# An eight-stage kernel on one core: fewer idle products in the last batch, squares in another place of ScalarE's list, own PSUM places for the last chunk

## The chip, the core and the metric

The kernel runs on one core of a Trainium2 chip. The core has a matrix engine (TensorE, PE in the profile), a vector engine (VectorE, DVE), a scalar engine (ScalarE, ACT), GpSimd (POOL), and SyncE (SP), which here only starts transfers (DMA) between HBM and SBUF. Each engine works through its own list of instructions in order; semaphores make one wait for another. The matrix engine writes to PSUM, which has 8 banks of 512 float32 for each of 128 partitions. The metric is the time of one execution on the device in microseconds; lower is better.

## What is computed

Cut to what matters:

```python
for t in range(S):                       # attention: B=4, H=8, S=768, D=48
    new_re = ar * S_re - ai * S_im       # a = (a_re, a_im), scaled to magnitude <= 0.999
    new_im = ar * S_im + ai * S_re
    S_re, S_im = new_re + outer(k[t], v[t]), new_im
    y[t] = q[t] @ S_re
x = y as [3072, 384]
logits = x @ phi                         # soft mixture of experts, 8 experts x 4 slots
d = softmax over tokens;  slot_input = d.T @ x
slot_out[e] = relu(slot_input[e] @ w1[e]) @ w2[e]
x = softmax over slots(logits) @ slot_out
out = relu(x @ w_in)**2 @ w_out          # second feed-forward, 2048 wide
```

## The kernel before

The recurrence is worked chunk by chunk: a batch has NC = 6 chunks of 128 steps, B = 4 batches, NT = 24 chunks. For a whole batch VectorE builds the running products of the decays `a` in the tile `big` (a scan: L798, L800, L804, then three block steps that end with L827, its copy L811 ahead of each). ScalarE and VectorE first bring `a` to its magnitude: squares (L381, L382), logarithms and exponentials, `inv_mag` (L404), `bend` (L410), then VectorE's `normalise` (L772). ScalarE's `sign_planes` (L448, L449, L451) makes negated copies of the imaginary plane; the scan of a batch opens with `init_products` (L782), which waits for the semaphores `signed` and `an_ready`. Behind the scan ScalarE takes the squares of the products (`product_squares`, L420, in two parts), VectorE adds them (`square_sums`, L833), and ScalarE makes logarithms and exponentials of them between two table loads (L430, L426, L433, L439).

For each chunk n VectorE makes weighted keys and queries (`key_query`, L894; `weigh`, L876) and a turn matrix (`build_turn`, L906); SyncE stacks them with six transfers (L269) into `stk`. On the matrix engine, iteration n of the main loop (the last lines of the kernel) runs: `scores(n)` (L1127), for every second n `flip` (L1207) of a pair of chunks, `outputs(n-1)` (L1167, L1170), `flip`, `next_state(n)` (L1145, L1148), `weighted_sums` of the pair (L1216, L1220), `turn_x(n-1)` (L1196), `logits(n-1)` (L1184). Between them stand idle products: `keep_busy(count)` (L1113) multiplies the identity into partitions 96 to 127 of PSUM bank 7, which nobody reads. VectorE masks the scores (`apply_mask`, L915), ScalarE copies results out of PSUM: `copy_kt` (L458), `copy_state` (L464), `copy_y` (L470), `copy_raw` (L477), `copy_x` (L485), the exponentials of a pair (L491, L497, L499), `copy_flipped` (L507), `copy_sums` (L511).

What sets the order: every engine's list is written out by hand. ScalarE's loop runs over batches p and chunks c; iteration (p, c) does the copies for chunk n = 6(p-1)+c and, between them, the preparation of batch p+1 (`inv_mag`, `bend` at c = 4, table loads and signs at c = 5). VectorE's loop has the same shape; `go` and `fill` put steps of the next batch's scan between the steps of the chunks. So iterations c = 4 and c = 5 are where a batch hands over to the next: "the hand-over" below. From chunk 18 on there is no next batch to prepare. Chunk 23 is the last; after it come the last pair's exponentials, flips and weighted sums, and then the experts (L1264 on) and the feed-forward (L1367 to L1397), 96 rounds that take the second half of the time. The experts' weights (`wt`) are loaded in halves by ScalarE's queue (L366, L372) and whole by SyncE's (L284, L290).

PSUM: scores fill banks 0 to 3, `s_ps` (states) and `lgt_ps` (logits) lie in bank 4, `y_ps` (outputs) in bank 5, `x_ps` and the flips in bank 6, the sums in bank 7.

## Time and profile before

| what | us |
|---|---|
| median of 3 runs | 618.05 |
| lowest, highest | 617.24, 618.3 |
| profiled execution, its time | 617.78 |
| its span (first to last instruction) | 616.1 |
| PE busy | 512.4 (83%) |
| VectorE busy | 392.4 (64%) |
| ScalarE busy | 339.4 (55%) |

The rows further down come from the profiled execution. Times in them are us from the start of its span. A row of a timeline gives start, length, engine, line of the kernel, operation, what is written from what, shapes, and in square brackets how long the engine sat idle before it and what released it. Rows of one line that follow one another are merged (x3); matmuls overlap, so the length of a matmul row is longer than the distance to the next row.

### The profile page before, as it was taken

What the parts mean: (1) busy time and instruction counts of PE and PEld (TensorE: products, weight loads), DVE (VectorE), ACT (ScalarE), POOL (GpSimd) and SP (SyncE); (2) the same over time, 40 slices, a digit from 0 to 9 for tenths busy, and PEclk for the clock granted to TensorE, in tenths of its full rate; (3) what the DMA queues carried; (4) which work ended last, traced back from release to release, by engine and by line L of the source; (5) the groups of instructions that cost most, each with busy time, mean ns of one, the idle gap of its engine ahead of it and who ended that gap; (6) DMA issues with size and microseconds to landing.
All of it is one profiled execution on the core that took longest, in us unless ns stands there. A gap on an engine that the chain in (4) does not pass through costs nothing.

```text
span 616.1 us, 11719 instructions
## 1 busy us (share of the span) xinstructions
PE 512.4 (83%) x4566; PEld 386.4 (63%) x4566; DVE 392.4 (64%) x649; ACT 339.4 (55%) x593; POOL 138.4 (22%) x118
## 2 busy tenths in 40 slices
PE   1000459995998869997999999999999999999997
PEld 1000147774667646775788644578888888888886
DVE  5899999979999799995353151599423333233322
ACT  6818714697456953375243412676655555555653
POOL 7000000000000000000000000266555555555553
PEclk9655589997999979997999999999999999999999
DMA  7400575647655358886799999200101001010101
GB/s 272 153 1 0 113 207 129 146 93 193 170 119 147 71 152 205 231 210 145 190 278 257 422 426 421 99 1 2 53 0 53 0 1 51 2 51 2 53 0 52
DMA packets 41319, 79.59 MB, mean 129 GB/s; under 512 B 7344, under 2 KB 28976, under 8 KB 40112
## 3 DMA queue, kind: packets, MB, share of 16 engines
q1 hardware_dynamic: 39104, 67.44, 38.3%
q10 hardware_dynamic: 2160, 11.40, 5.3%
q8 instruction: 36, 0.59, 0.4%
q14 instruction: 19, 0.16, 0.1%
HBM read 55.12 MB, written 4.72 MB: 97 GB/s over the span
## 4 chain that ended last, share of the span: by engine, by line
PE 61%; DVE 24%; ACT 5%; issue 5%; DMA 3%; SPq 2%; DVEq 0%; ACTq 0%
PE ps L1397 10%; PE ps L1393 10%; PE ps L1394 10%; PE ps L1127 7%; PE ps L1113 4%; DVE tt L798 4%; PE ps L1367 3%; DVE big L772 3%; DVE tt L800 3%; DVE big L804 3%; PE ps L1184 2%; PE ps L1170 2%; DMA stk<-xout 2%; PE ps L1167 2%; PE ps L1287 2%
## 5 line engine op out<-in xcount | busy, mean ns | idle before, releaser
L1092 DVE TENSOR_TENSOR qs<-rs 128x512 f32<-128x512 f32 x96 | 82.7, 861 | 118.8 <-ACT rs L674 118.8
L735 POOL TENSOR_TENSOR hlo<-qs,hhi 128x512 fp32r<-128x512 f32 x96 | 126.1, 1313 | 125.0 <-DVE qs L1092 119.8
L1113 PE MATMUL ps<-ident 128*32 128x512 bf16 x274 | 81.3, 408 | 52.7 <-DVE xout L894 52.7
L1393 PE MATMUL ps<-hhi,who 128*128 128x512 f32 x285 | 110.9, 389 | 0.0
L1394 PE MATMUL ps<-hhi,wlo 128*128 128x512 f32 x285 | 110.9, 389 | 0.0
L674 ACT ACTIVATE rs<-ps 128x512 f32<-128x512 f32 x96 | 57.4, 598 | 82.2 <-PE ps L1367 82.1
L1127 PE MATMUL ps<-stk 112*128 112x224 f32 (+1 forms) x384 | 77.8, 358 | 12.7 <-DMA stk<-xout 12.7
L1127 PEld LDWEIGHTS ps<-stk 112*128 112x128 f32 x384 | 69.5, 199 | 23.9 <-DMA stk<-xout 18.3
L1397 PE MATMUL ps<-hlo,who 128*128 128x512 f32 x285 | 80.5, 391 | 0.1
L727 POOL MEMSET sinz<- 128x768 f32 x1 | 0.7, 738 | 335.9 <-PE ps L1170 335.9
L1113 PEld LDWEIGHTS ps<-ident 128*32 128x32 bf16 x274 | 23.0, 100 | 77.7 <-DVE xout L894 53.0
L678 ACT ACTIVATE hhi<-rs 128x512 fp32r<-128x512 f32 x96 | 60.8, 633 | 3.1
L1397 PEld LDWEIGHTS ps<-hlo,who 128*128 128x128 f32 x285 | 53.2, 188 | 12.2 <-POOL hlo L735 1.3
L1393 PEld LDWEIGHTS ps<-hhi,who 128*128 128x128 f32 x285 | 53.5, 188 | 11.2
L1394 PEld LDWEIGHTS ps<-hhi,wlo 128*128 128x128 f32 x285 | 53.5, 188 | 11.1
L915 DVE TENSOR_TENSOR asb<-ps,mask 128x512 f32<-128x512 f32 x48 | 32.5, 686 | 28.7 <-ACT kts L458 14.5
L458 ACT ACTIVATE kts<-ps 128x384 f32<-128x384 f32 x40 | 19.5, 487 | 52.4 <-PE ps L1127 52.4
L894 DVE TENSOR_TENSOR xout<-big,xq 128x768 f32<-128x768 f32 x48 | 45.7, 953 | 0.5
L1367 PE MATMUL ps<-cst,ust 128*128 128x512 f32 x96 | 37.4, 392 | 0.2 <-DVE ust L1074 0.2
L1170 PE MATMUL ps<-asb,vr 128*48 128x128 f32 x384 | 35.5, 273 | 0.0
L1167 PE MATMUL ps<-stk,st 112*48 112x128 f32 x320 | 31.8, 276 | 0.0
L1184 PE MATMUL ps<-xts,phs 112*32 112x128 f32 x576 | 28.3, 294 | 3.4 <-issue 2.9
(152 smaller groups left out, 795.5 us busy)
## 6 DMA issues: line engine op xcount, KB each, us to landing
stk<-xout SPq DMA_DIRECT2D x144, 128.0 KB, 3.7
wt<-in_w SPq DMA_DIRECT2D x8, 1536.0 KB, 15.2
wt<-in_w ACTq DMA_DIRECT2D x14, 768.0 KB, 6.1
big<-in_a_all SPq DMA_DIRECT2D x12, 768.0 KB, 5.5
xq<-in_xq SPq DMA_DIRECT2D x24, 384.0 KB, 4.2
vr<-in_v_all SPq DMA_DIRECT2D x24, 192.0 KB, 4.1
out<-ost SPq DMA_DIRECT2D x5, 768.0 KB, 3.5
wins<-in_w_in SPq DMA_DIRECT2D x1, 3072.0 KB, 19.8
```

The source lines that it names most:

```text
L674: nc.scalar.activation(rs[:, i % NQS, :], ps[:, i % 2, :], ACT.Relu).then_inc(relu_ready, 1)
L678: nc.scalar.activation(hhi[:, i % NHS, :], rs[:, i % NQS, :], ACT.Square).then_inc(hi_ready, 1)
L735: pool.tensor_tensor(hlo[:, i % NHS, :], qs[:, i % NQS, :], hhi[:, i % NHS, :].bitcast(F32), ALU.subtract).then_inc(lo_ready, 1)
L894: dve.tensor_tensor(o, e, x, ALU.mult).then_inc(kq_ready, 1)
L1092: dve.tensor_tensor(qs[:, i % NQS, :], rs[:, i % NQS, :], rs[:, i % NQS, :], ALU.mult).then_inc(sq_ready, 1)
L1113: nc.tensor.matmul(ps[P - SL:P, bank, :], idb[:, 0:SL], idle, start=True, stop=True)
L1127: last = nc.tensor.matmul(ps[:, h // 2, h % 2 * SK:h % 2 * SK + cols], x[:, 0:CH], x[:, CH:CH + cols], start=True, stop=True)
L1170: last = nc.tensor.matmul(y, vr[:, n % NV, h * D:(h + 1) * D], asb[:, n % 2, h], start=(c == 0), stop=True)
L1367: nc.tensor.matmul(ps[:, i % 2, :], ust[:, f * P:(f + 1) * P], cst[:, t * TW:(t + 1) * TW], start=True, stop=True).then_inc(g_done, 1)
L1393: nc.tensor.matmul(accs[k], wh[k], hi, start=(f == 0), stop=False)
L1394: nc.tensor.matmul(accs[k], wl[k], hi, start=False, stop=False)
L1397: last = nc.tensor.matmul(accs[k], wh[k], lo, start=False, stop=(f == F2B - 1))
```

## The change

It has five parts, two of them small.

1. Idle products. In iterations 19 to 23 of the matrix engine's loop the idle products before `scores`, `outputs`, `weighted_sums` and `turn_x` are gone (5 + 5 + 3 + 5 = 18 products); iteration 18 keeps its 20 before `scores` and one before the others.
2. Squares and masks, for the hand-overs after batch preparation 0, 1 and 2 (p < 3). On ScalarE at c = 4 the first part's squares stand where `inv_mag` and `bend` stood, ahead of the pair's exponentials; `inv_mag`, the second part's squares and `bend` follow the copy of the state. On VectorE the first `square_sums` comes behind the masks of the chunk, not ahead of them (for p = 1 and 2).
3. The last chunk's outputs, logits, transpose and flips go to banks 0 to 3, which the masks have read by then. `outputs(23)` follows `outputs(22)` at once, both `logits` come before the last but one `weighted_sums`; the copy of the last outputs is split over ScalarE and VectorE, and VectorE takes over the copies of `x` for chunks 22 and 23 and of the sums of pair 10.
4. In the first batch the last third of `normalise` is split into the imaginary and the real half, and the signs wait for the imaginary half alone (`im_ready`).
5. Three quarters of the weight tile 6 are loaded at chunks 1, 3 and 5 of p = 2 by ScalarE's queue, the last quarter at chunk 18, in place of two halves at chunks 18 and 19.

```diff
-        et_ps = [ps[:, 6, NU * XR:NU * XR + 2 * SL]] * (NT - 1) + [ps[:, 4, 0:2 * SL]]
+        et_ps = [ps[:, 6, NU * XR:NU * XR + 2 * SL]] * (NT - 2) + [ps[:, 3, 0:2 * SL], ps[:, 4, 0:2 * SL]]
...
+        last_y = ps[:, 0, :].rearrange("p (u t) -> p u t", u=NU)
+        last_lgt = ps[0:SR, 1, 0:CH]
+        last_x = ps[:, 2, 0:NU * XR].rearrange("p (u r) -> p u r", u=NU)
...
-        LOADED = [48 if k == 5 else 32 if k in EARLY + [10] else 16 for k in range(2 * NX)]
+        LOADED = [64 if k == 6 else 48 if k == 5 else 32 if k in EARLY + [10] else 16 for k in range(2 * NX)]
...
             def sign_planes(b, t):
-                act.wait_ge(an_ready, DT * b + t + 1)
+                if b == 0 and t == DT - 1:
+                    act.wait_ge(im_ready, 1)
+                else:
+                    act.wait_ge(an_ready, DT * b + t + 1)
                 if b and t == 0:
...
                 act.wait_ge(y_done, m + 1)
                 if m >= 2:
                     act.wait_ge(x_done, m - 1)
+                if m == NT - 1:
+
+                    nc.scalar.activation(xts[0:D, m % 2], last_y[0:D], ACT.Copy).then_inc(last_y_copied, 1)
+                    return
                 nc.scalar.activation(xts[:, m % 2], y_ps, ACT.Copy).then_inc(y_copied, 1)
...
@@ -538,6 +551,9 @@
             for p in range(B + 1):
                 for c in range(NC + 2 * (p == B)):
                     n = (p - 1) * NC + c
+                    if p == B - 2 and c % 2:
+
+                        load_part(6, c // 2, c // 2 + 1)
...
                             magnitude(p + 1, 1)
                             log_mag(p + 1, 0)
                         elif c == 4:
-                            for t in range(DT):
-                                inv_mag(p + 1, t)
-                            for t in range(DT):
-                                bend(p + 1, t)
+                            product_squares(p, 0, 0)
+                            product_squares(p, 0, 1)
...
                             act.wait_ge(kq_ready, 2 * NC * (B - 1))
-                        load_half(NC + c)
+                        if c == 0:
+                            load_part(6, 3, 4)
+                        if c >= 2:
+                            load_half(NC + c)
...
                             magnitude(p + 1, 2)
                             log_mag(p + 1, 1)
-                    if p < B and c == NC - 2:
-
-                        product_squares(p, int(p == B - 1), 0)
-                        product_squares(p, int(p == B - 1), 1)
+                    if p == B - 1 and c == NC - 2:
+
+                        product_squares(p, 1, 0)
+                        product_squares(p, 1, 1)
...
@@ -614,19 +631,22 @@
                         elif c == 3:
                             log_mag(p + 1, 2)
                         elif c == 4:
+                            for t in range(DT):
+                                inv_mag(p + 1, t)
                             product_squares(p, 1, 0)
                             product_squares(p, 1, 1)
-                    if pair is not None:
+                            for t in range(DT):
+                                bend(p + 1, t)
+                    if pair is not None and n != NT - 1:
                         copy_sums(pair)
                     if p == B - 1 and c == NC - 2:
                         exponential(p, 0, 1)
                     if n == NT - 1:
                         copy_y(n)
-                    if n == NT:
-                        copy_raw(n - 1)
+
+                    if 1 <= n < NT - 1:
+                        copy_x(n - 1)
                     if 1 <= n <= NT:
-                        copy_x(n - 1)
-                    if 1 <= n < NT:
                         copy_raw(n - 1)
...
+                if b == 0 and t == DT - 1:
+
+                    for c, done in ((1, im_ready), (0, an_ready)):
+                        dve.scalar_tensor_tensor(out=grid(PL[0] + c * PF + t * PT, [1, PT]), in0=grid(U_ + t * PT, [1, PT]),
+                                                 scalar=KNEE, in1=grid(RAW + c * PF + t * PT, [1, PT]), op0=ALU.subtract,
+                                                 op1=ALU.mult, reverse0=True).then_inc(done, 1)
+                    return
...
-                    if 0 < p < B and c == NC - 1:
+                    if p == B - 1 and c == NC - 1:
 
                         one(p)
...
+            def last_copy_y():
+
+                dve.wait_ge(y_done, NT)
+                dve.wait_ge(x_done, NT - 2)
+                dve.tensor_copy(xts[R1:R1 + D, (NT - 1) % 2], last_y[R1:R1 + D]).then_inc(last_y_copied, 1)
...
+            def last_copy_x(m):
+                dve.wait_ge(x_done, m + 1)
...
+                x = bass.AP(ps, x.offset, [list(x.ap[0]), [XR, NU], [R1, 2], [1, D]])
+                dve.tensor_copy(xsb[:, m % NX3, 0:DM].rearrange("p (u r e) -> p u r e", u=NU, r=2), x).then_inc(x_copied, 1)
+
+            def last_copy_sums(j):
+                dve.wait_ge(sums_done, j + 1)
+                dve.tensor_copy(sums[0:SR, :], sums_ps).then_inc(sums_copied, 1)
+
+            last_copy_y()
             running_max(NT // 2 - 1)
+            last_copy_sums(NT // 2 - 2)
+            for m in (NT - 2, NT - 1):
+                last_copy_x(m)
...
-                if n:
+                if 0 < n < NT - 1:
...
             def logits(m):
 
-                pe.wait_ge(y_copied, m + 1)
+                if m == NT - 1:
+                    pe.wait_ge(last_y_copied, 2)
+                else:
+                    pe.wait_ge(y_copied, m + 1)
                 pe.wait_ge(s_copied, turns(min(m + 2, NT)))
-                if m:
+                if m == NT - 1:
+                    pe.wait_ge(masked, 2 * NT)
+                elif m:
                     pe.wait_ge(raw_copied, m)
...
-                pe.wait_ge(y_copied, m + 1)
-                if m:
+                if m == NT - 1:
+                    pe.wait_ge(last_y_copied, 2)
+                else:
+                    pe.wait_ge(y_copied, m + 1)
+                if m == NT - 1:
+                    pe.wait_ge(masked, 2 * NT)
+                elif m:
                     pe.wait_ge(x_copied, m)
...
                 pe.wait_ge(exp_done, m // 2 + 1)
-                pe.wait_ge(x_copied, m // 2 * 2 + (2 if m >= NT - 4 else 3))
-                if m == NT - 1:
+                if m < NT - 2:
+                    pe.wait_ge(x_copied, m // 2 * 2 + (2 if m >= NT - 4 else 3))
+                if m == NT - 2:
+                    pe.wait_ge(masked, 2 * NT)
+                elif m == NT - 1:
                     pe.wait_ge(raw_copied, NT)
...
                 full = n < NT - NC
+
+                rest = int(n <= NT - NC or n >= NT)
                 pair = pair_at(n)
                 if n < NT:
                     if n:
-                        keep_busy(20 if n == NT - NC else 6 if full else 1)
+                        keep_busy(20 if n == NT - NC else 6 if full else 0)
                     scores(n)
                 if pair is not None:
                     flip(2 * pair)
                 if 1 <= n < NT:
-                    keep_busy(1)
+                    keep_busy(rest)
                     outputs(n - 1)
+                if n == NT - 1:
+                    outputs(n)
                 if pair is not None:
                     flip(2 * pair + 1)
                 if n < NT and has_turn(n):
                     keep_busy(2 if full else 0)
                     next_state(n)
+                if n == NT - 1:
+
+                    logits(n - 1)
+                    logits(n)
                 if pair is not None:
-                    keep_busy(1)
+                    keep_busy(rest)
                     weighted_sums(pair)
-                if n == NT - 1:
-                    outputs(n)
-                if n == NT:
-                    logits(n - 1)
                 if 1 <= n <= NT:
-                    keep_busy(2 if full else 1)
+                    keep_busy(2 if full else rest)
                     turn_x(n - 1)
-                if 1 <= n < NT:
+                if 1 <= n < NT - 1:
                     logits(n - 1)
```

ScalarE's list at the first hand-over with chunks in flight (p = 1, c = 4; chunk 4). Before, from the reciprocals of the magnitudes to the copy of the sums:

```order
L404 ACTIVATE big<-big 128x768 x3
L410 ACTIVATE big<-big 128x768 x3
L491 ACTIVATE eb<-eb 32x256
L458 ACTIVATE kts<-ps 128x384
L507 ACTIVATE lgx<-ps 128x2x32
L458 ACTIVATE kts<-ps 128x384
L420 ACTIVATE big<-big 128x6x288 x2
L470 ACTIVATE xts<-ps 128x512
L507 ACTIVATE lgx<-ps 128x2x32
L464 ACTIVATE st<-ps 112x384
L420 ACTIVATE big<-big 128x6x96 x2
L511 ACTIVATE sums<-ps 96x385
```

and now (L425 is the squares, L409 `inv_mag`, L415 `bend`, L466 `copy_kt`, L482 `copy_y`, L472 `copy_state`, L504 the exponentials, L524 the sums):

```order
L425 ACTIVATE big<-big 128x6x288 x2
L504 ACTIVATE eb<-eb 32x256
L466 ACTIVATE kts<-ps 128x384
L520 ACTIVATE lgx<-ps 128x2x32
L466 ACTIVATE kts<-ps 128x384
L482 ACTIVATE xts<-ps 128x512
L520 ACTIVATE lgx<-ps 128x2x32
L472 ACTIVATE st<-ps 112x384
L409 ACTIVATE big<-big 128x768 x3
L425 ACTIVATE big<-big 128x6x96 x2
L415 ACTIVATE big<-big 128x768 x3
L524 ACTIVATE sums<-ps 96x385
```

The three L404 and three L410 have moved from ahead of the exponentials to behind the copy of the state; the squares L420 on 288 columns have moved the other way.

The matrix engine's list from the scores of chunk 23 to the last weighted sums. Before, from the outputs of chunk 23 on (L1167 and L1170 alternate above the first row, too):

```order
L1170 MATMUL ps<-asb,vr 48x128 x2
L1113 MATMUL ps<-ident 32x512
L1196 MATMUL ps<-ident,xts 128x112 x4
L1184 MATMUL ps<-xts,phs 32x128 x24
L1113 MATMUL ps<-ident 32x512
L1196 MATMUL ps<-ident,xts 128x112 x4
L1207 MATMUL ps<-ident,eb 128x64 x2
L1113 MATMUL ps<-ident 32x512
L1216 MATMUL ps<-sums,scale_diag 32x385
L1220 MATMUL ps<-xsb,lgx 32x385 x2
```

and now, from the flip that follows the outputs of chunk 23 (L1238 is the logits, L1255 the transpose of `x`, L1162 the idle product, L1269 the flip, L1278 and L1282 the weighted sums):

```order
L1269 MATMUL ps<-ident,eb 128x64
L1238 MATMUL ps<-xts,phs 32x128 x24
L1278 MATMUL ps<-sums,scale_diag 32x385
L1282 MATMUL ps<-xsb,lgx 32x385 x2
L1255 MATMUL ps<-ident,xts 128x112 x4
L1162 MATMUL ps<-ident 32x512
L1255 MATMUL ps<-ident,xts 128x112 x4
L1269 MATMUL ps<-ident,eb 128x64 x2
L1162 MATMUL ps<-ident 32x512
L1278 MATMUL ps<-sums,scale_diag 32x385
L1282 MATMUL ps<-xsb,lgx 32x385 x2
```

The logits of both chunks now stand ahead of a weighted sum that used to stand ahead of the outputs of chunk 23, and the two flips of the last pair stand behind the transpose of chunk 23 as before.

VectorE's list behind the last masks, now (L1050, L1061 and L1057 are new on this engine; L948 is the running maximum, which stood alone before):

```order
L942 TENSOR_TENSOR asb<-ps,mask 128x512 x2
L1050 COPY xts<-ps 48x512
L948 TENSOR_REDUCE eb<-eb 96x1
L1061 COPY sums<-ps 96x385
L1057 COPY xsb<-ps 128x384 x2
```

Behind it the three copies stand in a row, one to each of the sums and the two `x`.

## Rows read from the trace of the kernel before

**Rows 1.** Windows: length, then PE, PEld, DVE, ACT, POOL busy (x count), granted clock, DMA share, GB/s.

```profile
146.00:148.00 2.00, 1.32 (x10) 1.02 (x13) 1.93 (x5) 0.90 (x3) 0.00 (x0) 0.50 0.84 199
296.00:341.00 45.00, 45.00 (x695) 37.16 (x694) 19.53 (x27) 17.90 (x45) 0.00 (x0) 1.00 0.92 252
```

**Rows 2.** Timeline of ScalarE, hand-over from batch 1 to 2 (p = 1, chunks 4, 5).

```profile
122.51 2.30 ACT L404 ACTIVATE big<-big 128x768 f32<-128x768 f32 x3
...
126.91 0.49 ACT L491 ACTIVATE eb<-eb 32x256 f32<-32x256 f32 x1
...
128.26 3.18 ACT L420 ACTIVATE big<-big 128x1728 f32<-128x1728 f32 x2
...
132.31 0.49 ACT L464 ACTIVATE st<-ps 112x384 f32<-112x384 f32 x1 [0.27 <-PE ps L1148]
132.70 1.25 ACT L420 ACTIVATE big<-big 128x576 f32<-128x576 f32 x2
133.84 0.47 ACT L511 ACTIVATE sums<-ps 96x385 f32<-96x385 f32 x1
...
143.92 0.52 ACT L451 ACTIVATE big<-big 128x384 f32<-128x384 f32 x1
```

**Rows 3.** Timeline of VectorE, same hand-over.

```profile
131.47 1.96 DVE L833 TENSOR_TENSOR big<-big 128x1728 f32<-128x1728 f32 x1 [3.66 <-ACT big L420]
...
144.70 0.18 DVE L782 COPY a<-big 128x36 f32<-128x36 f32 x1
```

**Rows 4.** Timeline of the matrix engine, same hand-over.

```profile
127.46 0.27 PE L1207 MATMUL ps<-ident,eb 64*128 64x64 f32 x1 [1.07 <-ACT eb L491]
...
146.68 1.01 PE L1196 MATMUL ps<-ident,xts 112*128 112x112 f32 x4 [6.50 <-ACT xts L470]
...
151.06 3.29 PE L1127 MATMUL ps<-stk 112*128 112x224 f32 x16 [0.44 <-DMA stk<-xout]
```

**Rows 5.** Timelines of ScalarE and VectorE, hand-over from batch 2 to 3.

```profile
217.72 0.52 ACT L451 ACTIVATE big<-big 128x384 f32<-128x384 f32 x1
...
218.64 0.18 DVE L782 COPY a<-big 128x36 f32<-128x36 f32 x1
```

**Rows 6.** Timelines of ScalarE and VectorE, first batch and its hand-over.

```profile
21.73 0.52 ACT L448 ACTIVATE big<-big 128x384 f32<-128x384 f32 x1 [0.16 <-DVE big L772]
...
55.07 3.18 ACT L420 ACTIVATE big<-big 128x1728 f32<-128x1728 f32 x2 [0.40 <-DVE big L827]
...
60.75 1.28 ACT L430 ACT_TABLE_LOAD   x1
...
69.74 0.53 ACT L451 ACTIVATE big<-big 128x384 f32<-128x384 f32 x1
...
71.39 0.18 DVE L782 COPY a<-big 128x36 f32<-128x36 f32 x1
```

**Rows 7.** Timeline of the matrix engine in the last batch, around two idle products.

```profile
304.17 0.39 PE L1113 MATMUL ps<-ident 128*32 128x512 bf16 x1
304.26 0.50 PE L1184 MATMUL ps<-xts,phs 112*32 112x128 f32 x9
...
307.92 0.39 PE L1113 MATMUL ps<-ident 128*32 128x512 bf16 x1
308.24 1.08 PE L1170 MATMUL ps<-asb,vr 128*48 128x128 f32 x16
```

**Rows 8.** Timelines of the matrix engine and ScalarE, the last chunk's end.

```profile
342.99 0.39 PE L1113 MATMUL ps<-ident 128*32 128x512 bf16 x1
...
346.85 0.43 PE L1167 MATMUL ps<-stk,st 112*48 112x128 f32 x4
...
354.31 0.48 PE L1216 MATMUL ps<-sums,scale_diag 96*32 96x385 f32 x1
...
348.87 0.60 ACT L470 ACTIVATE xts<-ps 128x512 f32<-128x512 f32 x1 [1.42 <-PE ps L1170]
...
352.27 0.28 ACT L477 ACTIVATE eb<-ps 96x128 f32<-96x128 f32 x1 [1.26 <-PE ps L1184]
```

16 lines of the change are left out of this document (10 added, 6 removed).

## The prediction

> **What bounds the kernel now.** I read first the windows of the trace by stage, then the timelines of the three engines at the places where the diff edits a list, each time asking which wait ends last. Three kinds of stretch matter.
>
> In the last batch the matrix engine is the bound: from 296 to 341 it is busy 45.00 of 45.00 us, with a granted clock of 1.00 (2.4 GHz) [rows 1]. What is taken from its list there comes off the time, as long as nothing else is late next.
>
> At a hand-over between batches it is idle: 6.50 us pass before the transposes at 146.68, released by ScalarE's copy of the outputs (L470) [rows 4]. ScalarE is the engine to follow here. From 122.51 its list runs without a gap to speak of: reciprocals and bends, the pair's exponentials at 126.91, the squares at 128.26, the state at 132.31 after 0.27 idle, more squares, the sums at 133.84, and, through the two table loads, to the last sign at 143.92 [rows 2]. VectorE waits 3.66 us for the squares in the middle (L833), and that also holds the masks behind it; but it opens the next scan (L782, which needs all signs) at 144.70, when the last sign ended at 144.44 [rows 2, 3]. So both engines come out at the same moment, and whichever gets longer decides.
>
> Inside batches 1 to 3 VectorE's scan sets the pace (scores wait for the stack transfer of what VectorE made: 0.44 us at 151.06 [rows 4]). A scan that opens later shifts the whole batch behind it, because every wait of the matrix engine, ScalarE's copies and VectorE's masks hangs on the same transfers.
>
> **The squares and masks, ScalarE's side.** The edit swaps what ScalarE does in two of its waiting times. Before: 4.40 us of reciprocals and bends (122.51 to 126.91) lie beside the scores, and the 3.1 us of first squares lie beside the outputs of chunk 3. Now the squares lie beside the scores, from 122.51 to 125.6; their input, the second block step, was done before. Nothing at all lies beside the outputs and the next state, and the 4.40 us come behind the state copy. Step by step at the hand-over 1 to 2:
>
> The flip started at 127.46 because the exponentials were late, after 1.07 us of idling [rows 4]. Now it comes some 1.15 us earlier (the idle time plus an end of a modelled product), and so do outputs and next state. The state copy, which waited for next state until 132.31 [rows 2], starts at 131.16 and takes the 0.39 up to the squares, until 131.55. Then 4.40 of reciprocals and bends and 1.14 of second squares (132.70 to 133.84) follow: the sums start at 131.55 + 4.40 + 1.14 = 137.09, not at 133.84. ScalarE is 3.25 us late. It has bought 1.15 us and lost some 4.4 us of cover. From there its list is as before, so the last sign ends at 147.7.
>
> **The same place, VectorE's side.** The wait of 3.66 us goes [rows 3]. What is late next: the first sum no longer waits, but the second needs the second squares, which end at 134.9 by the working above (137.09 less the bends, half of 4.40). Keys and queries of the next batch could come at most 2.5 us earlier (3.66 less some 1.2 for the masks that now stand first); with the wait for the second squares I estimate 0.9. `weigh` then needs an exponential that ScalarE makes 3.2 us later, and L782 needs the signs: 147.7 against 144.70, so **+3.0 us** for the scan (3.25 less the 0.26 between 144.44 and 144.70). The transposes behind L470 are 3.2 us late as well; there the 0.44 us of idle before the scores of chunk 6 is used up first, +2.8 [rows 4]. The scan's figure is the larger, and it carries through the batch.
>
> Hand-over 2 to 3 is the same list one batch on. The last sign ended at 218.24, L782 ran at 218.64 [rows 5], so 0.40 of ScalarE's 3.2 is hidden: **+2.8**.
>
> Hand-over 0 to 1 has no chunks in flight. ScalarE had finished the bends and waited 0.40 us for the second block step until 55.07 [rows 6]. Now it has nothing to do before that. From 54.9 (0.16 earlier, see below) it does squares 3.1, reciprocals and bends 4.40, second squares 1.14, and reaches the table load at 63.5, not 60.75: 2.75 late. The signs end at 73.0, not 70.27, and L782 had run at 71.39 [rows 6]: **+1.6**.
>
> Sum of part two: 1.6 + 3.0 + 2.8 = **+7.4 us**. Its lower bound is a gain, if ScalarE's lateness never reached VectorE: twice the 0.9 above. Its upper bound is 2.75 + 3.25 + 3.2 = 9.2. I take the working, because L782's wait for the signs is in the code and both sides of it have their rows.
>
> **First batch.** The last signs started at 21.73, only 0.16 us after ScalarE had become free [rows 6]. Whatever the half-sized `normalise` gains, 0.16 is all that ScalarE can use. It is counted above (54.9), with nothing to add.
>
> **Idle products, 18 of them.** Their price is not one number. Before the outputs one costs 0.32 us, from 307.92 to 308.24 [rows 7]; iterations 19 to 22 lose one each there, and a product after another kind of product needs some start of its own, so I take 0.30: 1.2 us. Before scores it costs nothing: at 304.17 it starts ahead of the last nine logits at 304.26 [rows 7], since it writes partitions 96 to 127 and they write 0 to 95. The weighted sums write 0 to 95 as well, so I count nothing there and nothing for the transpose behind them. That leaves the transposes of iterations 19 and 21; the logits behind these also wait for the state copy, which is late next, so 0.2 each, 0.4. Sum **-1.6** (bounds: -1.0, and 18 times 0.32, -5.8; I stay near the low end, since eight of the rows' kind are hidden).
>
> The Trainium skill ("TensorE: Matmul & The Clock Gate", Part 3, on row and column tiling) says that small products at different tile positions overlap in the array but start and end strictly in program order. By the second half an idle product queued behind the logits could not start before the last of them, and would cost its own length each time, some 0.2 us for eight of them, 1.6 us more gain. The first row of [rows 7] stands ahead of the second, which speaks for the overlap and against that price.
>
> **The last chunk.** Outputs of chunk 23 started at 346.85. Now they follow those of chunk 22, which can start at 342.99, where an idle product stood, and take about 1.8: 344.8. The copy that ran at 348.87 would run at 346.8, but on ScalarE the flipped pair's copy now comes between: 347.1, done at 347.7. Before, the copy of the last logits followed 3.40 us after it (348.87 to 352.27); now only the 1 us of logits(23) lies between: 348.85. From there to the last weighted sums it was 2.04 us (352.27 to 354.31), which would give 350.9 [rows 8]. But other things end later: the matrix engine still has a weighted sum, two transposes and an idle product to do (about 2.2 us, until 350.9), and VectorE's last `x` copy waits for the second transpose and ends near 351.6. So 354.31 becomes 351.6: **-2.7**. Its bounds: -2.0 (the outputs' shift alone) and -3.4 (350.9). No row shows VectorE copying 48 or 96 partitions from PSUM; the nearest is ScalarE's 0.60 for 512 columns [rows 8]. From 0.3 to 0.7 each, three in a row, moves the end by 0.6 either way.
>
> **Weight tile 6.** It adds three issues on ScalarE's queue in batch 2, none on a path that waits. Their transfers share the DMA engines with the stacks that scores wait for. At 199 GB/s [rows 1] 384 KB is 2.0 us; if the stacks of two chunks stood behind one each, that is 4.0, and it is 0 if the slack ahead of the masks takes it. I take **+0.2**. In the last batch it takes load off the DMA engines, share 0.92 [rows 1], and the matrix engine shows no wait there that it could give back: 0.
>
> **Sum.** 7.4 + 0.2 - 1.6 - 2.7 = **+3.3 us**. The profiled execution took 617.78, 0.27 below the median of the runs; laid on the median, 618.05 + 3.3 = 621.35, **621.3 us**. The experts and the feed-forward behind this are as before.
>
> **Rivals.**
> (a) The masks are the path, and ScalarE's lateness is not (the scan opens late, but VectorE has room). Then part two gives 2 x 0.9 back and the time is 618.05 - 1.8 - 1.6 - 2.7 + 0.2 = 612.2. For it: the 3.66 us wait [rows 3]. Against: 144.44 beside 144.70 [rows 2, 3]. It decides if ScalarE's late list stays under 0.26 us. Chance 0.10.
> (b) The scan opens late, but half of it is given back in the batches, because the matrix engine and not VectorE sets some chunks' pace: 3.7 in place of 7.4, 617.65. Chance 0.18. For it: the wait at 151.06 is just 0.44.
> (c) The last chunk gains nothing, since VectorE's three copies, one behind the other, take the place of the removed waits: 623.9. Chance 0.08.
> (d) Without idle products the matrix engine pauses in the last batch and its clock falls. After the 6.50 us pause the granted clock was 0.50 (1.2 GHz), and four transposes lasted 1.01 us [rows 1, 4]. Against: nothing else but useful products is left in a stretch without idle time, and the new waits are tenths. If a quarter of the 45 us came to run at half clock, it would take 11 us more: 632. Chance 0.03. The Trainium skill (same page, Part 1, on what is happening) has the throttled state as the default that activity releases, which is the rule against removing idle products; it can bite only where real products do not fill the time.
>
> **Chances and range.** The forecast has 0.61, and (a) to (d) 0.39. What a measurement of this kernel can tell from no change is about 0.2%, 1.2 us. The forecast's own spread is 619 to 623.5, and about 0.05 of its 0.61 falls within 0.2%; of (b), 0.10 falls within and 0.08 below. Slower: 0.56 + 0.08 + 0.03 = 0.67; within: 0.15; faster: 0.18. The range has to take in (b) and (c): 616.3 to 624.4.
>
> **What would show it.** Right: ScalarE idles 1.5 us twice between the second `copy_kt` and the state copy of chunks 4 and 10; the copy that opens each scan (now L809) waits for signs at all three hand-overs; the matrix engine idles some 10 us before the transposes of chunk 4, not 6.50; from scores(19) to the last weighted sums 4.3 us less. Wrong: VectorE's scan of batch 2 opening at or before 144.7 (then (a)), a first scores of batch 3 shifted by less than half of the sum (then (b)), a granted clock under 1.00 after chunk 19 (then (d)).

## The result and the profile after

| | before | changed |
|---|---|---|
| median of 6 runs, us | 617.30 | 621.54 |
| lowest, highest | 616.49, 618.30 | 620.57, 625.29 |
| profiled execution, its span | 617.78, 616.1 | 620.58, 618.8 |

The ratio is 1.0074, with a 95% interval of 1.0046 to 1.0103: the changed kernel is slower, by 4.2 us in the medians and by 2.8 us between the two profiled executions. The forecast was 621.3. It fell on the measured number, but two of its terms were wrong and offset each other, as the experiments show. (The ratios leave out executions over 1.5% above the fastest of the same kernel; the medians are of all, so the two can differ a little.)

Code lines have moved: L782 is now L809, L833 L860, L420 L425, L404 L409, L410 L415, L451 L459, L470 L482, L1127 L1176, L1167 L1216, L1196 L1255.

**Hand-overs.** ScalarE of the changed kernel, hand-over 1 to 2 (start, length, engine, line; in brackets the idle time before, and who ended it); answers [rows 2]:

```profile
123.94 3.17 ACT L425 ACTIVATE big<-big 128x1728 f32<-128x1728 f32 x2
...
130.28 0.60 ACT L482 ACTIVATE xts<-ps 128x512 f32<-128x512 f32 x1 [1.62 <-PE ps L1219]
...
132.59 0.49 ACT L472 ACTIVATE st<-ps 112x384 f32<-112x384 f32 x1 [1.60 <-PE ps L1197]
132.98 2.30 ACT L409 ACTIVATE big<-big 128x768 f32<-128x768 f32 x3
135.18 1.24 ACT L425 ACTIVATE big<-big 128x576 f32<-128x576 f32 x2
136.32 2.30 ACT L415 ACTIVATE big<-big 128x768 f32<-128x768 f32 x3
138.52 0.47 ACT L524 ACTIVATE sums<-ps 96x385 f32<-96x385 f32 x1
...
148.53 0.52 ACT L459 ACTIVATE big<-big 128x384 f32<-128x384 f32 x1
```

The squares now lie beside the scores, and ScalarE then stands idle 1.62 and 1.60 us for the matrix engine with nothing left to put there. Reciprocals and bends come behind. The sums start at 138.52, 4.68 later than at 133.84 [rows 2]; 1.43 of that the batch brought along (its chunk 4 started that much later), so 3.25 were made here.

VectorE of the changed kernel, same hand-over and the two others; answers [rows 3, 5, 6]:

```profile
72.91 0.18 DVE L809 COPY a<-big 128x36 f32<-128x36 f32 x1 [1.72 <-ACT big L459]
...
136.45 0.76 DVE L860 TENSOR_TENSOR big<-big 128x576 f32<-128x576 f32 x1 [2.87 <-ACT big L425]
...
149.08 0.18 DVE L809 COPY a<-big 128x36 f32<-128x36 f32 x1 [1.72 <-ACT big L459]
...
225.40 0.18 DVE L809 COPY a<-big 128x36 f32<-128x36 f32 x1 [1.72 <-ACT big L459]
```

The wait of 3.66 us ahead of the first sum became one of 2.87 ahead of the second, and each scan opens behind a wait of 1.72 us for signs. Against 71.39, 144.70 and 218.64 [rows 3, 5, 6] the scans open 1.52, 4.38 and 6.76 us later. Before the transposes of a hand-over the matrix engine now waits longer, here from batch 2 to 3, where it was 6.49 us (10.82 at the hand-over 1 to 2, where it was 6.50 [rows 4]):

```profile
227.61 1.01 PE L1255 MATMUL ps<-ident,xts 112*128 112x112 f32 x4 [10.83 <-ACT xts L482]
```

**Last batch.** Windows from one chunk's first scores to the next one's, chunks 18 to 22 (length, then PE, PEld, DVE, ACT, POOL busy, granted clock, DMA share, GB/s), of the changed kernel; they answer the second of [rows 1]:

```profile
301.59:310.61 9.02, 9.02 (x121) 7.17 (x120) 4.54 (x6) 3.27 (x8) 0.00 (x0) 1.00 0.70 170
310.61:317.99 7.38, 7.28 (x127) 6.57 (x124) 4.54 (x7) 2.83 (x6) 0.00 (x0) 1.00 0.98 247
317.99:328.69 10.70, 9.50 (x152) 7.80 (x149) 5.38 (x8) 4.72 (x13) 0.00 (x0) 1.00 0.84 219
328.69:336.95 8.26, 8.16 (x140) 7.45 (x140) 3.68 (x5) 2.56 (x5) 0.00 (x0) 1.00 0.75 221
336.95:346.37 9.42, 9.42 (x151) 7.80 (x148) 1.38 (x2) 4.45 (x12) 0.00 (x0) 1.00 0.94 299
```

The same stretches of the kernel before:

```profile
295.67:304.69 9.02, 9.02 (x121) 7.17 (x120) 4.55 (x6) 3.28 (x8) 0.00 (x0) 1.00 0.62 181
304.69:312.54 7.85, 7.85 (x130) 6.72 (x127) 4.96 (x7) 2.83 (x6) 0.00 (x0) 1.00 0.98 262
312.54:322.33 9.79, 9.79 (x155) 7.89 (x153) 4.55 (x6) 4.45 (x12) 0.00 (x0) 1.00 1.07 268
322.33:331.06 8.73, 8.73 (x146) 7.61 (x143) 4.09 (x6) 2.83 (x6) 0.00 (x0) 1.00 1.00 254
331.06:340.81 9.75, 9.75 (x156) 7.90 (x153) 1.38 (x2) 4.45 (x12) 0.00 (x0) 1.00 0.91 285
```

Read the second column of times, PE busy: without idle products a chunk from 19 on needs 0.57, 0.29, 0.57 and 0.33 less. The length shrinks by 0.47, 0.47 and 0.33 in chunks 19, 21 and 22, but it grows by 0.91 in chunk 20, where 1.20 us of the window is no work at all:

```profile
328.69 1.59 PE L1176 MATMUL ps<-stk 112*128 112x224 f32 x7 [1.20 <-DMA stk<-xout]
```

The scores of chunk 21 wait for their stack to land. I had not foreseen this wait. It also spoils one of the prediction's signs: from scores(19) to the last weighted sums it took 46.44 us, 49.62 before, 3.2 less and not 4.3. The last chunk came out as worked out, here the matrix engine's outputs(23) and last weighted sums, and ScalarE's copy of the last logits; answers [rows 8]:

```profile
350.35 0.39 PE L1216 MATMUL ps<-stk,st 112*48 112x128 f32 x4
...
357.05 0.51 PE L1278 MATMUL ps<-sums,scale_diag 96*32 96x385 f32 x1
...
354.42 0.27 ACT L489 ACTIVATE eb<-ps 96x128 f32<-96x128 f32 x1 [0.60 <-PE ps L1238]
```

**The sum in the trace.** Scan of batch 3 +6.76; scores of chunk 18 only +5.92 (0.84 given back on the way, see the clock below); scores of chunk 23 +5.56; last weighted sums 357.05 against 354.31 [rows 8], +2.74; the executions +2.80.

### The profile page after: what moved, and what is told of

It reads as the page before. It is cut to its first block, busy times and chain, and to the rows that moved or that the text cites. A ratio compares the mean times of both kernels' runs of the same rounds, so it can differ in the third digit from the quotient of the medians.

```text
span 618.8 us, 11687 instructions
## 1 busy us (share of the span) xinstructions
PE 506.3 (82%) x4548; PEld 384.7 (62%) x4548; DVE 395.1 (64%) x654; ACT 338.2 (55%) x590; POOL 138.5 (22%) x118
## 4 chain that ended last, share of the span: by engine, by line
PE 66%; DVE 13%; ACT 11%; DMA 4%; issue 4%; SPq 2%; ACTq 0%; DVEq 0%
PE ps L1463 11%; PE ps L1459 10%; PE ps L1460 10%; PE ps L1176 8%; PE ps L1162 5%; PE ps L1433 4%; DMA stk<-xout 3%; DVE tt L825 3%; DVE big L831 3%; DVE tt L827 3%; PE ps L1219 2%; PE ps L1216 2%; PE ps L1238 2%; SPq L274 2%; PE ps L1353 2%
## 5 line engine op out<-in xcount | busy, mean ns | idle before, releaser
L1162 PE MATMUL ps<-ident 128*32 128x512 bf16 x256 | 73.4, 404 | 52.4 <-DVE xout L921 52.4
L1176 PE MATMUL ps<-stk 112*128 112x224 f32 (+1 forms) x384 | 76.8, 355 | 16.6 <-DMA stk<-xout 16.6
L1176 PEld LDWEIGHTS ps<-stk 112*128 112x128 f32 x384 | 68.6, 196 | 27.3 <-DMA stk<-xout 20.7
L1162 PEld LDWEIGHTS ps<-ident 128*32 128x32 bf16 x256 | 21.2, 99 | 75.7 <-DVE xout L921 52.7
L466 ACT ACTIVATE kts<-ps 128x384 f32<-128x384 f32 x40 | 19.5, 487 | 49.8 <-PE ps L1176 49.8
L1255 PE MATMUL ps<-ident,xts 112*128 112x112 f32 x96 | 15.3, 284 | 21.8 <-ACT xts L482 21.8
L1216 PE MATMUL ps<-stk,st 112*48 112x128 f32 x320 | 31.8, 276 | 0.0
```

The costliest lines, as they stand in the source:

```text
L1162: nc.tensor.matmul(ps[P - SL:P, bank, :], idb[:, 0:SL], idle, start=True, stop=True)
L1176: last = nc.tensor.matmul(ps[:, h // 2, h % 2 * SK:h % 2 * SK + cols], x[:, 0:CH], x[:, CH:CH + cols], start=True, stop=True)
```

## Experiments

The five parts are called idle products, squares (with the masks), last chunk, normalise, and tile 6, as in the change. The runs of 1 to 4 shared the same runs of the kernel before (median 618.1), so did 5 to 8 (617.8) and 9 to 12 (618.6); each of these three groups ran on a chip of its own, so that ratios are compared between groups, and not medians. In these hours the kernel before spread from 613.8 to 627.7, so that intervals are some 0.3% to either side, and differences of 1 us are not settled. The diffs are cut to what matters.

**1. The changed kernel with the squares as before.** Against the changed kernel:

```diff
                         elif c == 4:
-                            product_squares(p, 0, 0)
-                            product_squares(p, 0, 1)
+                            for t in range(DT):
+                                inv_mag(p + 1, t)
+                            for t in range(DT):
+                                bend(p + 1, t)
...
-                    if p == B - 1 and c == NC - 2:
+                    if p < B and c == NC - 2:
...
-                    if p == B - 1 and c == NC - 1:
+                    if 0 < p < B and c == NC - 1:

                         one(p)
```

> The changed kernel with the squares and masks put back as they were (ScalarE's list at the hand-overs, VectorE's first sum of squares before the masks); idle products, last chunk, weight tile 6 and the halved normalise stay as changed. Theory (ScalarE's late list holds back the scan, 1.5 + 2.9 + 2.4 = 6.8 us in the trace of the changed kernel): the time falls from 621.5 to about 614.7, or to 615.7 if the 1.2 us that the changed kernel got back at the last hand-over goes too; scans 1 to 3 open at 71.4, 144.7 and 218.6 again, give or take 0.5. Rival (the new waits come from the other parts, the DMA traffic of weight tile 6 or the pauses without idle products, and the squares only move a wait): under 3 us of the 6.8 come back, the time stays above 618.5, and scans 2 and 3 open over 1.5 us later than in the kernel before.

Median 615.0, ratio to the kernel before 0.9931 (0.9899 to 0.9963). Scans 1 to 3 opened at 71.18, 145.22 and 218.98, within 0.52 of the kernel before. Against the changed kernel's 1.0074 this is 1.4% or about 9 us (6 to 11 with both intervals; the medians differ by 6.5). That agrees with the 6.8 expected, and not with the rival's 3. In the trace the third scan opened 6.42 us earlier than in the changed kernel. The rest of the change, on its own, gains.

**2. The kernel before with the squares alone.** The same lines as in experiment 1, the other way round, in the kernel before.

> The kernel before with the squares and masks alone moved. Theory: 617.3 + 6.8 = 624.1, the scans opening at 72.9, 149.1 and 225.4; 623.1 if the last hand-over gives back some 1.0 us as it did in the changed kernel. Rival (as for the run with the squares put back): under 620.

Median 626.5, ratio 1.0150 (1.0114 to 1.0185), 7.0 to 11.4 us. The scans opened at 73.39, 149.81 and 226.21, the last one 7.57 late. The profiled execution took 624.4, 6.6 more than that of before. The theory stands; the times show rather more than the trace.

**3. The kernel before with the last chunk alone.**

```diff
                 if 1 <= n < NT:
                     keep_busy(1)
                     outputs(n - 1)
+                if n == NT - 1:
+                    outputs(n)
...
+            last_copy_y()
             running_max(NT // 2 - 1)
+            last_copy_sums(NT // 2 - 2)
```

> The kernel before with the last chunk alone changed. Theory: the whole saving of 2.8 us between scores(23) and the last weighted sums belongs to this part: 614.5 (scan openings unchanged). Rival (it needs the free slots where the idle products stood, or VectorE's three new copies in a row take the gain): 615.8 or more.

Median 614.8, ratio 0.9965 (0.9940 to 0.9990), 0.6 to 3.7 us less. From the first scores of chunk 23 to the last row of weighted sums it took 11.35 us, 13.91 before: 2.56 gained (2.88 together with the idle products gone from these iterations). So the part works alone. The profiled execution took 618.45 all the same: it was 2.0 us ahead of the kernel before at scores(20) and 3.3 behind at scores(23). scores(21) had waited 3.54 us for its stack, and the chunk behind took 1.70 us longer than before. Its code up to there is that of the kernel before; why it waited is taken up behind the experiments.

**4. The kernel before without the 18 idle products.**

```diff
+                rest = int(n <= NT - NC or n >= NT)
...
-                        keep_busy(20 if n == NT - NC else 6 if full else 1)
+                        keep_busy(20 if n == NT - NC else 6 if full else 0)
...
-                    keep_busy(1)
+                    keep_busy(rest)
                     outputs(n - 1)
```

> The kernel before with 18 idle products of the last batch removed, nothing else. Theory (each removed one is worth 0.2 to 0.3 us where it stood before outputs or a transpose, nothing where it overlapped; 1.6 us in all, of which the changed kernel lost 1.2 to a stack transfer that chunk 21's scores then waited for): between 615.7 and 616.9, with a wait of the matrix engine for a stack transfer in the last batch if it is the upper figure. Rival 1 (idle products are never overlapped, each costs its own length): 3.2 us less, 614.1, and 2 us or more gained between scores(19) and scores(23). Rival 2 (the clock falls without them): granted clock under 1.00 after scores(19), 620 or more.

Median 621.9, ratio 1.0037 (0.9998 to 1.0075): no gain, and more likely a loss of some 2 us. My figure is out, and so is rival 1's. Rival 2 had named both the time and a lower clock, but the trace shows another cause than the one it gave. Matrix engine and windows of chunks 20 and 21:

```profile
323.23 4.98 PE L1127 MATMUL ps<-stk 112*128 112x224 f32 x16 [3.90 <-DMA stk<-xout]
```

```profile
309.85:323.23 13.38, 9.48 (x151) 7.79 (x149) 5.37 (x8) 4.72 (x13) 0.00 (x0) 1.00 1.08 248
323.23:333.19 9.96, 9.86 (x141) 8.82 (x141) 3.67 (x5) 2.56 (x5) 0.00 (x0) 0.83 0.57 168
```

The DMA engines are full in chunk 20 (share 1.08), scores(21) waits 3.90 us, and after that wait the granted clock of the next chunk is 0.83, with the scores at 4.98 us where they take 3.29 at full clock ([rows 4], third row). That chunk took 9.96 us, 1.70 more than the 8.26 of the changed kernel. Up to the wait the clock was 1.00 without the idle products, and experiment 3, which kept them, lost as much in the same place. So the product count was right (chunks 19 and 22 were 0.46 and 0.34 shorter), and 3.90 + 1.70 were lost between.

That is not all of this execution's loss. At the last weighted sums it was 1.45 us behind the kernel before, at its end 5.4: it lost 4.0 in the experts, where it ran at half the clock. Windows of experiment 4, then of the kernel before:

```profile
355.00:360.00 5.00, 4.43 (x22) 2.72 (x23) 0.30 (x2) 1.04 (x5) 0.00 (x0) 0.50 1.00 424
360.00:365.00 5.00, 5.00 (x28) 2.56 (x30) 3.92 (x8) 0.84 (x1) 0.29 (x1) 0.50 1.01 428
```

```profile
355.00:360.00 5.00, 4.42 (x39) 2.64 (x38) 2.62 (x5) 0.72 (x2) 0.29 (x1) 1.00 1.01 428
360.00:365.00 5.00, 5.00 (x49) 2.22 (x45) 3.18 (x6) 1.80 (x3) 0.00 (x0) 1.00 1.00 419
```

The code there is the same in both, and no run shows what set the clock there. In the traces of experiments 6 and 8 the clock fell in the same place too, for 1.7 us more; in the other eleven it stayed at 1.00. One execution therefore can't divide the 2 us of the medians among these causes.

**5. The changed kernel with tile 6 loaded as before.**

```diff
-                    if p == B - 2 and c % 2:
-
-                        load_part(6, c // 2, c // 2 + 1)
...
-                        if c == 0:
-                            load_part(6, 3, 4)
-                        if c >= 2:
-                            load_half(NC + c)
+                        load_half(NC + c)
```

> The changed kernel with weight tile 6 loaded as before (two halves in the last batch). The runs so far showed stack transfers as what the last batch waits for: scores(21) waited 3.5 and 3.9 us in the two kernels that had one part of the change without the moved weight tile, and 1.2 and 1.4 us in the two that had it moved; after a wait of 3.5 us or more the granted clock of the next chunk was 0.84, which cost 1.5 us more. New theory: the moved weight tile is worth some 3 to 4 us as soon as the matrix engine gets to scores(21) earlier, so here the time rises from 621.5 to 624.5 or more, with scores(21) waiting over 2.5 us for its stack and a granted clock under 0.9 in the chunk behind it. Rival (my forecast: its load costs 0.2 and saves nothing): 621.3, the wait at scores(21) stays near 1.2.

Median 625.7, ratio 1.0126 (1.0091 to 1.0161). The changed kernel had 1.0074: tile 6 moved is worth 0.5%, about 3 us (0.4 to 6), in this company. Matrix engine and windows of chunks 20 and 21:

```profile
333.18 6.26 PE L1170 MATMUL ps<-stk 112*128 112x224 f32 x16 [5.00 <-DMA stk<-xout]
```

```profile
318.69:333.18 14.49, 9.49 (x152) 7.80 (x149) 5.38 (x8) 4.72 (x13) 0.00 (x0) 0.97 1.09 238
333.18:344.42 11.24, 11.14 (x141) 9.74 (x141) 3.68 (x5) 2.56 (x5) 0.00 (x0) 0.73 0.42 134
```

Wait and clock are both there: 5.00 us where the changed kernel waited 1.20, then 0.73. The rival is out.

**6. The kernel before with tile 6 alone moved.** The lines of experiment 5, the other way round, in the kernel before.

> The kernel before with weight tile 6 alone moved. New theory: the median falls by 1 to 2 us, since some executions of the kernel before must pay the wait at scores(21) too (its times spread from 615 to 625), and the spread narrows; DMA share of the chunk ahead of scores(21) 0.85 in place of 1.07. My forecast's view: 0.2 slower.

Median 619.2, ratio 1.0023 (0.9993 to 1.0053). No gain by itself; the expectation was wrong. In the trace the relief is there (the stack lands 7.39 us after the start of scores(20), 9.74 before), but there is a price that I had missed. ScalarE of this kernel around the issue at chunk 7:

```profile
161.77 3.05 ACTq L372 DMA_DIRECT2D wt<-in_w  x1
164.93 0.84 ACT L381 ACTIVATE big<-big 128x768 f32<-128x768 f32 x1 [2.89 <-issue]
```

The issue took 3.05 us, where one takes 0.33 in the last batch, and nothing behind it on ScalarE's list can start. The copy of the outputs came 0.92 us later than before, but the scan of batch 3 opened only 0.18 later (218.82), so this trace doesn't show that the issue cost the kernel time.

**7. Last chunk, normalise and tile 6; squares as before, idle products kept.** Against experiment 1 it has `keep_busy(1)` where that has `keep_busy(rest)`, and 1 where that has 0:

```diff
-                        keep_busy(20 if n == NT - NC else 6 if full else 0)
+                        keep_busy(20 if n == NT - NC else 6 if full else 1)
...
-                    keep_busy(rest)
+                    keep_busy(1)
```

> The kernel with the last chunk, weight tile 6 and the halved normalise changed, the squares as before and the idle products of the last batch kept. It differs from the first experiment by the 18 idle products alone. New theory (with the stack transfer as the bound ahead of scores(21), a removed idle product only lengthens that wait; behind chunk 21 some 0.8 us are left): 0 to 0.8 us above the first experiment's time in the same hours, so 615.0 to 615.8. Rival (they are worth the 1.6 us of my sum): 616.6.

Median 613.4, ratio 0.9937 (0.9900 to 0.9973), against 615.0 and 0.9931 in experiment 1. The expected 615.0 to 615.8 was missed, since this group ran faster than experiment 1's. By the ratios the removal of the idle products gains 0.4 us, from 2.6 of loss to 3.4 of gain with both intervals, so the times don't rule out the rival's 1.6. The traces speak against it: from scores(18) to scores(23) it took 45.10 us with the products and 45.04 without them, where scores(21) waited 1.45. Here it had no wait.

**8. The kernel before without idle products, and tile 6 moved.** The diffs of experiments 4 and 6 together.

```diff
+                    if p == B - 2 and c % 2:
+
+                        load_part(6, c // 2, c // 2 + 1)
...
-                        keep_busy(20 if n == NT - NC else 6 if full else 1)
+                        keep_busy(20 if n == NT - NC else 6 if full else 0)
```

> The kernel before with the idle products of the last batch removed and weight tile 6 moved. The idle products alone gave 621.9 against 618.1. New theory (that loss is the wait for the stack of chunk 21 and the lower clock behind it, and the moved weight tile takes most of both away): 616.0 to 617.5, the wait at scores(21) 1 to 2 us, clock 1.00 behind it. Rival (the loss comes from the missing idle products themselves, by the clock or by the order on the matrix engine): it stays over 620.

Median 616.8, ratio 0.9986 (0.9957 to 1.0015), against 1.0037 without the moved tile: 0.5% or 3 us (0.2 to 6) once more. Window of chunk 20, and the wait behind it:

```profile
312.94:325.01 12.07, 9.48 (x151) 7.79 (x148) 5.37 (x8) 4.73 (x13) 0.00 (x0) 1.00 0.86 215
```

```profile
325.01 1.21 PE L1133 MATMUL ps<-stk 112*128 112x224 f32 x5 [2.59 <-DMA stk<-xout]
```

DMA share 0.86 in place of 1.08, the wait 2.59 in place of 3.90, and no loss of clock behind it: chunk 21 took 8.28 us. The wait was longer than the 1 to 2 us expected. This profiled execution took 620.7, almost the longest of its twelve, so the time and the trace are not of a piece. ScalarE in batch 2 of this kernel shows the price again:

```profile
160.86 2.37 ACTq L372 DMA_DIRECT2D wt<-in_w  x1
...
170.22 0.84 ACT L381 ACTIVATE big<-big 128x768 f32<-128x768 f32 x1 [3.50 <-DMA big<-in_a_all]
```

The raw amplitudes for the next batch landed late as well: ScalarE waited 3.50 us for them, the copy of the outputs behind was late, and the scan of batch 3 opened at 220.08, 1.44 later than [rows 5].

**9. The kernel before with ScalarE's half of the squares.** The ScalarE lines of experiment 1's diff, the other way round; VectorE's sum stays ahead of the masks.

> The kernel before with ScalarE's half of the squares part alone (first squares beside the scores, reciprocals and bends behind the state copy); VectorE still makes its first sum of squares ahead of the last masks. Theory (ScalarE's list is what holds the scan, VectorE's half adds or saves little): the scans open 1.5 to 2, 4.4 to 5 and 6.8 to 7.6 us later than in the kernel before, and the time is that of the second experiment within its noise, 624.5 to 626.5. Rival (the price comes from both halves together, by masks that stand ahead of the sum): the third scan opens less than 5 us later, 623 or less.

Median 626.4, ratio 1.0114 (1.0081 to 1.0147). The scans opened 1.87, 3.93 and 6.22 us late. It is ScalarE's half that costs. VectorE's half costs nothing on top (experiment 10). The second and third figures are 0.5 and 0.6 under the ranges that I gave, and the third is 1.35 under the 7.57 of experiment 2: in the trace the masks ahead may cost some more, in the times nothing that can be told.

**10. The kernel before with VectorE's half.**

```diff
-                    if 0 < p < B and c == NC - 1:
+                    if p == B - 1 and c == NC - 1:

                         one(p)
```

> The kernel before with VectorE's half alone: the last masks stand ahead of the first sum of squares in batches 1 and 2. Theory (the scan's opening waits for ScalarE's signs, 0.26 and 0.40 us behind which VectorE is ready anyway, so a shorter VectorE list gives nothing): scans open within 0.3 us of the kernel before, time within 1 us of it, 617.0 to 618.5. Rival (a) of the prediction (the masks are the path): 1.8 us faster, 616.0.

Median 617.4, ratio 0.9964 (0.9936 to 0.9992). VectorE of this kernel, hand-over 1 to 2:

```profile
131.47 1.96 DVE L833 TENSOR_TENSOR big<-big 128x1728 f32<-128x1728 f32 x1 [2.31 <-ACT big L420]
...
144.47 0.18 DVE L782 COPY a<-big 128x36 f32<-128x36 f32 x1 [0.89 <-ACT big L451]
```

The masks took 1.3 us of the wait, as meant, and the sum still stands at 131.47, the same as in [rows 3]. The scans opened at 144.47 and 218.34, 0.23 and 0.30 earlier than in the kernel before, and 0.23 this execution was ahead from the first scan on. The trace shows no gain for rival (a); the times lie 0.5 to 4 us under the kernel before, for which I have no place in the trace. It stays open.

**11. Experiment 6, the quarters issued at chunks 3, 4, 5 of the pass.**

```diff
-                    if p == B - 2 and c % 2:
+                    if p == B - 2 and c >= NC - 3:

-                        load_part(6, c // 2, c // 2 + 1)
+                        load_part(6, c - NC + 3, c - NC + 4)
```

> The kernel before with weight tile 6 moved, but its first three quarters issued at chunks 3, 4 and 5 of the third pass in place of 1, 3 and 5. In the runs with chunk 1, that issue took ScalarE 2.4 to 3.2 us (another one takes 0.33), and the raw amplitudes behind it in the same DMA engines landed later: ScalarE waited 0.5 to 3.5 us for them. Theory (this is why the moved tile alone showed no gain, 619.2 against 617.8): the issue takes under 1 us again, the copy of the outputs that follows comes 1 to 2 us earlier, and the median is 616 to 617.5, 2 us under that of the sixth experiment. Rival (the moved tile gives nothing without the other parts, wherever it is issued): 618 to 619.5.

Median 618.1, ratio 1.0026 (0.9992 to 1.0060), the same as 1.0023 in experiment 6. In the trace the first of the moved issues takes 0.39 us and not 3.05, so that part of the theory holds. The copy of the outputs after chunk 7 is at 167.78, 1.9 us earlier than in experiment 6 (169.69), and the scan of batch 3 at 218.10, 0.7 earlier than in experiment 6; the times show nothing of it, and the 616 to 617.5 expected was missed. By them the rival holds: the moved tile gives nothing without the other parts.

**12. Experiment 7 with the quarters issued as in 11.** The same edit.

> What the experiments point to: last chunk and halved normalise changed, weight tile 6 moved with its parts at chunks 3, 4 and 5, squares and masks as before, idle products kept. Theory: 0.5 to 1.5 us under the seventh experiment's 613.4, so 612 to 613, 9 us under the changed kernel and 5 under the kernel before, with no wait over 0.5 us for a stack transfer in the last batch. Rival (the place of the issue doesn't matter): 613.4 or more.

Median 614.1, ratio 0.9937 (0.9901 to 0.9972), the very ratio of experiment 7. The 612 to 613 expected was missed: where the issue stands makes no difference that can be measured. scores(21) waited 0.86 us here, more than I gave. Experiments 1, 7 and 12 are the three fastest versions, by 0.6 to 0.7% than the kernel before and 1.4% than the changed one; their intervals don't tell them apart.

## Why the prediction came out as it did

| term | forecast | in the trace | in the times |
|---|---|---|---|
| squares | +7.4 | +6.8 (scan of batch 3) | +9.3 (7.0 to 11.4), +7.0 (5.0 to 9.1) ScalarE's half |
| idle products | -1.6 | -1.6 of work, +1.2 of wait | +2.3 (-0.1 to 4.6) alone |
| last chunk | -2.7 | -2.8 | -2.2 (-3.7 to -0.6) alone |
| tile 6 | +0.2 | waits 1.2 in place of 5.0 (experiment 5) | -3 in company, +1.4 (-0.4 to 3.3) alone |
| clock at the last hand-over | none | -0.8 | |

(The column of times is the ratio less 1, times 618.)

**Squares: right, by its own steps.** ScalarE idles 1.62 and 1.60 us, the sums are 3.25 late (forecast 3.25), the scan of batch 2 opens 2.86 later than its start alone would give (3.0), that of batch 1 1.52 (1.6), that of batch 3 2.38 (2.8). L809 waits for signs at all three. Experiments 1, 2 and 9 show that ScalarE's list is the cause. Rival (a) is out: with VectorE's order unchanged the scan was 6.2 late. Rival (b) too: 5.92 of the 6.76 were still there at chunk 18.

**Normalise: within the forecast.** The wait of 0.16 us [rows 6] is gone; more than that can't be told from one execution to the next.

**Last chunk: right.** outputs(23) at 350.35 less the 5.56 of its batch is 344.8 (344.8), the raw copy 348.86 (348.85), the last weighted sums 351.5 (351.6). Rival (c) is out by experiment 3.

**Idle products: the count was right, the term wrong.** The four chunks lost 1.56 us (0.47, 0.29, 0.47, 0.33), as costed, and the price of one behind logits was indeed nothing beyond that. What failed is the clause "as long as nothing else is late next". The stack of chunk 21 is, and the trace of the kernel before had this already. SyncE's last transfer of that stack there, and in the same view the time from issue to landing:

```profile
315.67 0.61 SPq L269 DMA_DIRECT2D stk<-xout  x1
DMA to landing us min/median/max: 6.6/6.6/6.6
```

It landed at 322.3, and scores(21) started at 322.33: there was no slack (0.04 us by the trace's exact times). In chunk 20 the DMA engines were already full, which I read only as a mean: share 0.92 over 45 us [rows 1], where the window of chunk 20 has 1.07. The first of the six transfers is issued 6.95 to 6.96 us after the start of scores(19) in all 14 traces, so what is saved before scores(19) moves the stack along. The 0.47 + 0.29 saved between scores(19) and scores(21) doesn't, and becomes wait. With it the sum closes: the stack took 11.08 us from its first issue to its landing in the changed kernel, 10.64 before, and 0.76 + 0.44 - 0.04 is 1.16, measured 1.20. Where the wait is long the clock falls too, which is rival (d)'s mechanism with another trigger and another price: not the missing idle products by themselves (clock 1.00 from scores(18) to the last weighted sums in the changed kernel) but the waits of 3.54, 3.90 and 5.00 us, and 1.7 to 3.0 us, not 11. The Trainium skill ("TensorE: Matmul & The Clock Gate", Part 1, on oscillation in real kernels) describes a loop in which each wait for the next slice of data throttles the engine again. Experiments 3, 4 and 5 agree: 0.84, 0.83 and 0.73 after waits of 3.54, 3.90 and 5.00 us, and 1.00 after 1.20 and 2.59.

**Tile 6: wrong, and the largest error.** The step was "the matrix engine shows no wait there that it could give back: 0". No wait says only that the slack is not negative. What decides at scores(21) is when the stack lands. Its last transfer is issued just ahead of a weight half from ScalarE's queue, which is issued 3.62 us after the start of scores(20) in every trace. Times here are us after that start; the matrix engine is ready for scores(21) at 9.8, or at 9.5 without the idle products:

| kernel | idle products | tile 6 | last transfer ahead of the weight half by, us | stack landed at | wait at scores(21) |
|---|---|---|---|---|---|
| before | kept | late | 0.50 | 9.74 | 0 |
| 10 | kept | late | 0.60 | 10.11 | 0.34 |
| 9 | kept | late | 0.77 | 10.50 | 0.73 |
| 2 | kept | late | 1.31 | 10.12 | 0.35 |
| 3 | kept | late | 0.23 | 13.30 | 3.54 |
| 4 | gone | late | 0.24 | 13.34 | 3.90 |
| 5 | gone | late | 0.14 | 14.44 | 5.00 |
| 6 | kept | moved | 0.64 | 7.39 | 0 |
| 12 | kept | moved | 0.47 | 10.62 | 0.86 |
| 7 | kept | moved | 0.40 | 8.53 | 0 |
| 11 | kept | moved | 0.57 | 10.68 | 0.91 |
| 1 | gone | moved | 0.06 | 10.89 | 1.45 |
| 8 | gone | moved | -0.01 | 12.03 | 2.59 |
| changed | gone | moved | 0.11 | 10.65 | 1.20 |

Two things go with a late landing. One is tile 6 left in the last batch: with the last transfer under 0.25 us ahead the stack lands at 13.3 to 14.4 with it and at 10.7 to 12.0 without. The other is that nearness itself: with tile 6 late it sets 13.3 to 14.4 apart from 9.7 to 10.5. Without the idle products chunk 19 is 0.46 shorter, so the stack is issued that much later against scores(20), and its last transfer falls within 0.24 us of the weight half in all five such kernels, in one of nine with the products. How early the matrix engine gets to scores(19) doesn't decide: it was 2.68 us early in experiment 6 without a wait, and 6.62 late in experiment 5 with the longest. These are single executions, so each row is a sample, and no run moved that one weight half: that the nearness is a cause is read from the rows and not tested. The ratios of 4 against 8 and of 5 against the changed kernel give about 3 us for tile 6 in company of removed idle products, each with an interval from near 0 to 6. In the traces of 4 and 8 the stack landed 1.31 us sooner with the tile moved. The Trainium skill ("DMA: Bandwidth & Descriptors", "Issuing engines are not separate DMA queues") says that transfers issued from different engines share the same 16 DMA engines and interleave. The trace agrees: the halves are issued from ScalarE's queue, and with them in the last batch the stacks, which SyncE issues, landed up to 3.8 us later (5.00 against 1.20).

**So the sum held by luck.** The forecast's -1.6 + 0.2 for idle products and tile 6 stands against -0.4 in the trace of the changed kernel (5.92 less 5.56), where the moved tile kept the wait at 1.20. The last hand-over gave 0.8 back, squares were 0.6 under the forecast, and the last chunk 0.1. Between the profiled executions that makes 2.8, and the forecast was 3.3. What the last hand-over gave back is no merit of the change: the trace of the kernel before was one of three in 14 with the slowest clock there (see below). The other 1.4 us by which the medians differ more than the executions profiled have no place in a trace; the changed kernel's profiled execution was all but the quickest of its six.

The forecast's rival (c) adds up to 624.0 and not 623.9, which changes nothing.

**What the forecast should have had:** the interval above, once squares and last chunk are settled, hangs on tile 6. Without it the same change is at 625.7, outside the range of 616.3 to 624.4.

## What to carry to other kernels

A wait of zero is no slack of zero: before work is taken off the engine that sets the pace, find when each of its inputs lands, chunk by chunk and not in the mean, above all where the DMA engines are full. Here the trace of the kernel before would have said it: the stack landed 0.04 us ahead of its use. Work that fills another engine's waiting time is only free at the place where that wait is; of 4.4 us moved out from under such a wait, 1.5 to 2.9 came onto the path at each of three hand-overs. And parts of a change that only look neutral may pay for the others, so they are tested in company, not alone.
